# More buffers for the first pairs of attention, and a later start of a folded weight, in a fused retention and feed-forward kernel

## The reference

```python
scores = scale * np.matmul(q, k.transpose(0, 1, 3, 2))
Dmat = np.where(rel >= 0, gamma[:, None, None] ** rel[None, :, :], 0.0)
attn = np.matmul(scores * Dmat[None, :, :, :], v)
x = attn.transpose(0, 2, 1, 3).reshape(4608, 512)
h = np.maximum(np.maximum(x @ w1, x @ w2), x @ w3) @ w_out      # 512 -> 768 -> 512
return (((h @ u1) * (h @ u2)) @ u3) @ u_out                     # 512 -> 1024 -> 1024 -> 512
```

## Time and profile before

| | |
|---|---|
| median of three runs | 1245.4 us (1242.52 to 1248.57) |
| profiled execution | 1245.86 us, span 1244.1 us |
| PE busy | 1221.9 us, 98% of the span |
| DVE, ACT, POOL busy | 62%, 39%, 35% |
| attention (to the end of PE's values at 178.9 us) | 14% of the span |
| mean granted TensorE clock | 0.998 |

### The profile page before, as it was taken

The page is one execution under the profiler, slowest core; times in us unless marked ns, Lnnn a source line. Parts: engine busy times, 40 slices in busy tenths (PEclk is TensorE's granted clock), DMA queues, the critical chain, the costliest instruction groups (busy, mean ns, idle before and its releaser), DMA issues.

```text
span 1244.1 us, 21154 instructions
## 1 busy us (share of the span) xinstructions
PE 1221.9 (98%) x8288; PEld 1205.7 (97%) x8288; DVE 769.4 (62%) x1192; ACT 486.1 (39%) x779; POOL 435.3 (35%) x228
## 2 busy tenths in 40 slices
PE   7999999999999999999999999999999999999999
PEld 6999989999999999998999999999999999999998
DVE  6666857754546364657799668453545467875563
ACT  3433544423223232325555544242424243554441
POOL 2635529220100102051798562202020217265540
PEclk9999999999999999999999999999999999999999
DMA  9999954020302112052555541312131343444441
GB/s 341 331 328 333 309 166 159 33 96 27 102 27 82 46 56 72 27 171 80 198 202 190 171 155 55 109 52 102 51 109 57 109 153 125 153 152 160 152 159 65
DMA packets 88084, 169.96 MB, mean 137 GB/s; under 512 B 9904, under 2 KB 59184, under 8 KB 87984
## 3 DMA queue, kind: packets, MB, share of 16 engines
q1 hardware_dynamic: 87984, 168.60, 38.8%
HBM read 106.70 MB, written 61.87 MB: 135 GB/s over the span
## 4 chain that ended last, share of the span: by engine, by line
PE 85%; DVE 6%; DMA 3%; POOL 2%; issue 2%; SPq 1%; ACT 1%; DVEq 0%; ACTq 0%; POOLq 0%
PE ps L1075 25%; PE ps L1076 25%; PE ps L1077 25%; DVE wlo L807 2%; PE ps L975 2%; DVE clo L807 2%; PE ps L1023 2%; PE ps L1012 2%; POOL wraw L565 1%; DMA hd<-h 1%; PE ps L1038 1%; DMA xd<-xst 1%; PE ps L996 1%; PE ps L1042 1%; PE ps L1040 1%
## 5 line engine op out<-in xcount | busy, mean ns | idle before, releaser
L1075 PE MATMUL ps<-chi,whi 128*128 128x384 f32 x2016 | 675.4, 335 | 9.0 <-DVE h L897 6.4
L1077 PE MATMUL ps<-chi,wlo 128*128 128x384 f32 x2016 | 674.1, 334 | 0.0
L1076 PE MATMUL ps<-clo,whi 128*128 128x384 f32 x2016 | 674.0, 334 | 0.0
L565 POOL TENSOR_TENSOR raw<-raw,raw 128x768 f32<-128x768 f32 (+2 forms) x96 | 267.4, 2804 | 591.9 <-DMA raw<-xd 221.5
L1075 PEld LDWEIGHTS ps<-chi,whi 128*128 128x128 f32 x2016 | 378.9, 188 | 12.5 <-DVE h L897 8.3
L1076 PEld LDWEIGHTS ps<-clo,whi 128*128 128x128 f32 x2016 | 379.0, 188 | 0.0
L1077 PEld LDWEIGHTS ps<-chi,wlo 128*128 128x128 f32 x2016 | 378.8, 188 | 0.0
L807 DVE TENSOR_TENSOR clo<-raw,chi 128x768 fp32r<-128x768 f32 (+2 forms) x168 | 247.5, 1501 | 22.8 <-ACT chi L723 22.8
L723 ACT CAST chi<-raw 128x768 fp32r<-128x768 f32 (+2 forms) x168 | 180.5, 1081 | 85.1 <-PE ps L1077 61.7
L797 ACT COPY w<-ps 128x384 f32<-128x384 f32 x126 | 60.5, 480 | 249.8 <-PE ps L1077 248.3
L779 ACT COPY u<-ps 128x384 f32<-128x384 f32 x126 | 60.7, 482 | 159.2 <-PE ps L1077 155.8
(11 more groups left out here) (43 smaller groups left out, 838.5 us busy)
## 6 DMA issues: line engine op xcount, KB each, us to landing
qks<-qk SPq DMA_DIRECT2D x32, 576.0 KB, 6.5
gd<-h SPq DMA_DIRECT2D x96, 192.0 KB, 1.9
raw<-gd SPq DMA_DIRECT2D x24, 768.0 KB, 6.1
hd<-h SPq DMA_DIRECT2D x72, 192.0 KB, 1.9
raw<-hd SPq DMA_DIRECT2D x24, 576.0 KB, 5.7
x2d<-h SPq DMA_DIRECT2D x48, 192.0 KB, 2.4
raw<-x2d SPq DMA_DIRECT2D x24, 384.0 KB, 4.8
outT<-h SPq DMA_DIRECT2D x48, 192.0 KB, 1.9
```

Of the source, the lines that this page charges most:

```text
L565: return nc.gpsimd.tensor_tensor(out_, a, b, op)
L1075: nc.tensor.matmul(to, w1, x1, start=(start and k == 0), stop=False, skip_group_check=True)
L1076: nc.tensor.matmul(to, w1, x2, start=False, stop=False, skip_group_check=True)
L1077: last = nc.tensor.matmul(to, w2, x1, start=False, stop=(k == KH[st] - 1), skip_group_check=True)
```

## The change

Pairs 0 to 3 get buffers of their own for keys and state, and pairs 0 to 5 for queries and keys of the scores, in space that the second stage's weights use only later. More of the early loads therefore wait for nothing. In step 1 PE sums the state of each pair right after its scores (pair 3 in the PSUM bank of the folded weight), and DVE makes the state of pair 2 between the decays of pairs 2 and 3; in step 2 the state sums stand ahead of the queries. The folded weight begins in step 4: two quarters in steps 4 to 13, four in 14 to 16, and its loads, splits and reads move with it, some into places behind other loads of the same step. From pair 4 on the values of two pairs come in one load, and the tails of the values are loads of their own, two pairs each, for which PE waits before `values`. DVE clears four state buffers in place of two.

The diff, cut where it only puts `qk_buf(n)`, `k_buf(n)`, `v_buf(n)` or `state_buf(n)` in the place of a remainder, makes the buffers, or gives their semaphore counts:

```diff
-WC_FROM = 3
-QUARTERS = 4 * FT2
+QUARTERS = [0] * 4 + [2] * 10 + [4] * 3
...
+def qk_buf(n):
+    return n if n < 6 else n % 4
...
+def k_buf(n):
+    return n if n < 4 else n % 2
...
+def v_sem(n):
+    return n if n < 4 else (n - n % 2) % 6
...
+def state_buf(n):
+    return n if n < 4 else n % 2
...
-U3_LOAD = {min(2 * kb + WC_FROM - 2, STEPS - 3): kb for kb in range(FT2)}
-U3_SPLIT = {min(2 * kb + WC_FROM - 1, STEPS - 2): kb for kb in range(FT2)}
-UO_LOAD = {1: (0, 1), 2: (2, 3)}
-UO_SPLIT = {2: (0, 1), 3: (2, 3)}
-WC_READ = {min(2 * kb + WC_FROM + 1, STEPS - FT2 + kb): kb for kb in range(FT2)}
+U3_LOAD = {1: 0, 4: 1, 6: 2, 8: 3, 10: 4, 12: 5, 14: 6, 15: 7}
+U3_SPLIT = {3: 0, 5: 1, 7: 2, 9: 3, 11: 4, 13: 5, 14: 6, 15: 7}
+UO_LOAD = {2: (0, 1), 3: (2, 3)}
+UO_SPLIT = {3: (0, 1), 4: (2, 3)}
+WC_READ = {5: 0, 7: 1, 9: 2, 11: 3, 13: 4, 14: 5, 15: 6, 16: 7}
...
             def load_qk(n):
-                if n >= 4:
+                if n >= 6:
                     sp.wait_ge(scored, n - 3)
                     sp.wait_ge(q_decayed, n - 3)
...
+            def load_two_v(m):
+                n = 2 * m
                 if n >= 6:
-                    sp.wait_ge(valued, n - 5)
...
+                    sp.wait_ge(valued, n - 4)
+                sp.dma_start(vs[:, v_buf(n):v_buf(n) + 2, 0:NC * CH], vv[n:n + 2, :, :].rearrange("n p c -> p n c")
+                             ).then_inc(v_loaded[v_sem(n)], 16)
+
+            def load_tails(m):
+                n = 2 * m
+                sp.dma_start(vs[TAIL:P, v_buf(n):v_buf(n) + 2, NC * CH:], vt[n:n + 2, :, :].rearrange("n p c -> p n c")
+                             ).then_inc(vt_loaded[m % 3], 16)
...
             def load_k(n):
-                if n >= 2:
+                if n >= 4:
                     sp.wait_ge(state_summed, n - 1)
...
             load_v(1)
             load_k(1)
+            sp.dma_start(qtab[:, :, :], qdecay).then_inc(qtab_loaded, 16)
             load_qk(2)
-            sp.dma_start(qtab[:, :, :], qdecay).then_inc(qtab_loaded, 16)
+            load_decay(2, slice(4, HEADS))
+            load_k(2)
+            load_v(2)
             load_qk(3)
-            load_decay(2, slice(4, HEADS))
-            load_v(2)
+            load_k(3)
             load_v(3)
+            load_tails(0)
+            load_qk(4)
+            load_qk(5)
+            load_tails(1)
             for m in range(STEPS):
...
+                if m >= 2:
+                    if m in U3_LOAD:
+                        load_u3(U3_LOAD[m])
+                    if m in P1_W_LOAD:
+                        load_weight(P1_W_LOAD[m])
+                if m:
+                    for n in made_in(m + 1):
+                        load_k(n)
+                    if m in UO_LOAD:
+                        load_uo(UO_LOAD[m][0])
+                    for n in made_in(m + 2):
+                        load_qk(n)
+                    if m in UO_LOAD:
+                        load_uo(UO_LOAD[m][1])
+                    elif m == 1:
+                        load_u3(U3_LOAD[m])
+                if 2 * m + 4 < NP:
+                    load_two_v(m + 2)
+                    load_tails(m + 2)
+                for n in (2 * m - 2, 2 * m - 1):
+                    if n >= PAIRS:
+                        store_x(n)
...
             def make_state(n):
                 p = n % PAIRS
-                bank = S_WC if n == 1 else S_STATE
-                dve.wait_ge(state_summed, n + 2 - n % 2 if n >= 2 else n + 1)
+                bank = S_WC if n in (1, 3) else S_STATE
+                dve.wait_ge(state_summed, n + 2 - n % 2 if n >= 4 else n + 1)
...
             for m in range(STEPS):
                 for n in made_in(m):
                     decay_scores(n)
-                    if n == 0:
+                    if n in (0, 2):
                         make_state(n)
...
             def values(n):
                 pe.wait_ge(decayed, 3 * (n - n % 2 + 2))
+                pe.wait_ge(vt_loaded[n // 2 % 3], 16 * (n // 6 + 1))
...
             for m in range(STEPS):
                 for n in made_in(m):
                     scores(n)
-                    if m == 0:
+                    if m < 2:
                         sum_state(n)
                 for i in quarters(m):
                     wc_quarter(i)
+                for n in made_in(m) if m == 2 else ():
+                    sum_state(n)
                 for n in read_in(m):
                     query_state(n)
-                for n in made_in(m) if m else ():
+                for n in made_in(m) if m > 2 else ():
                     sum_state(n)
```

More of the change, by code:

```diff
@@ L177, in quarters, with qk_count, k_count, v_buf @@
 def quarters(m):
-    if m >= STEPS - 2:
-        return range(QUARTERS - 4 * (STEPS - m), QUARTERS - 4 * (STEPS - m) + 4)
-    return range(2 * (m - WC_FROM), 2 * (m - WC_FROM) + 2) if m >= WC_FROM else ()
-U3_LOAD = {min(2 * kb + WC_FROM - 2, STEPS - 3): kb for kb in range(FT2)}
-U3_SPLIT = {min(2 * kb + WC_FROM - 1, STEPS - 2): kb for kb in range(FT2)}
-UO_LOAD = {1: (0, 1), 2: (2, 3)}
-UO_SPLIT = {2: (0, 1), 3: (2, 3)}
-WC_READ = {min(2 * kb + WC_FROM + 1, STEPS - FT2 + kb): kb for kb in range(FT2)}
+    return range(sum(QUARTERS[:m]), sum(QUARTERS[:m + 1]))
+assert len(QUARTERS) == STEPS and sum(QUARTERS) == 4 * FT2
+def qk_buf(n):
+    return n if n < 6 else n % 4
+def qk_count(n):
+    return 16 if n < 6 else 16 * (n // 4 + (n % 4 > 1))
+def k_buf(n):
+    return n if n < 4 else n % 2
+def k_count(n):
+    return 16 if n < 4 else 16 * (n // 2)
+def v_buf(n):
+    return n % 6
+def v_sem(n):
+    return n if n < 4 else (n - n % 2) % 6
+def v_count(n):
+    return 16 if n < 4 else 16 * (n // 6 + 1)
+def state_buf(n):
[5 more added lines that the diff above has]
+WC_READ = {5: 0, 7: 1, 9: 2, 11: 3, 13: 4, 14: 5, 15: 6, 16: 7}
 P1_W_LOAD = {8: 0, 9: 1}
@@ L293, in build @@
         o += 2 * NC * CH * 4
-        state = [at(f"state{i}", [P, NC, P], f32, o + i * NC * P * 4) for i in range(2)]
+        state = [at(f"state{i}", [P, NC, P], f32, o + i * NC * P * 4 if i < 2 else first_at + (i - 2) * NC * P * 4)
+                 for i in range(4)]
+        first_at += 2 * NC * P * 4
+        assert first_at <= w_base[2]
         o += 2 * NC * P * 4
@@ L838, in make_state @@
                         if c == 0:
-                            nc.vector.tensor_copy(state[n % 2][own, c, own], new).then_inc(state_made, 1)
+                            nc.vector.tensor_copy(state[state_buf(n)][own, c, own], new).then_inc(state_made, 1)
                         else:
@@ L842, in make_state @@
                             nc.vector.scalar_tensor_tensor(
-                                state[n % 2][own, c, own], state[n % 2][own, c - 1, own], CHUNK_DECAY[2 * p + h], new,
-                                ALU.mult, ALU.add).then_inc(state_made, 1)
+                                state[state_buf(n)][own, c, own], state[state_buf(n)][own, c - 1, own],
+                                CHUNK_DECAY[2 * p + h], new, ALU.mult, ALU.add).then_inc(state_made, 1)
             def split_weight(wi, part):
@@ L974, in scores @@
                         keys = SEQ + c * CH
-                        nc.tensor.matmul(ps[:, 2 * (n % 2) + h, c * CH:(c + 1) * CH], qks[n % 4][own, keys:keys + CH],
-                                         qks[n % 4][own, c * CH:(c + 1) * CH],
+                        nc.tensor.matmul(ps[:, 2 * (n % 2) + h, c * CH:(c + 1) * CH], qks[qk_buf(n)][own, keys:keys + CH],
+                                         qks[qk_buf(n)][own, c * CH:(c + 1) * CH],
                                          start=(c == 0), stop=(c == NC - 1), skip_group_check=True)
@@ L1011, in query_state @@
                     bank, cols = x_cols(n, c)
-                    last = nc.tensor.matmul(ps[:, bank, cols], state[n % 2][:, c - 1, :],
+                    last = nc.tensor.matmul(ps[:, bank, cols], state[state_buf(n)][:, c - 1, :],
                                             qdec[n % 2][:, c - 1, 0:min(CH, SEQ - c * CH)],
@@ L1022, in values @@
                         own = slice(h * DH, h * DH + DH)
-                        last = nc.tensor.matmul(ps[own, bank, cols], vs[n % 6][:, c * P + h * DH:c * P + h * DH + DH],
+                        last = nc.tensor.matmul(ps[own, bank, cols], vs[:, v_buf(n), c * P + h * DH:c * P + h * DH + DH],
                                                 probs[n % 4][:, h, c * CH:min(SEQ, (c + 1) * CH)],
```

68 lines of the change are left out of this document (29 added, 39 removed).

## The result

The changed kernel takes 1260.8 us (median of five runs, 1257.7 to 1262.1) against 1245.4: 1.0117 of the time before, with a 95% interval of 1.0102 to 1.0132. It is some 15 us slower, where I forecast 1 us and allowed 5. The profiled execution took 1262.07 us for a span of 1260.3.

What follows compares the result with a forecast made beforehand. TensorE, busy 98% of the span, was taken to bound the kernel. The terms summed to +1.2 us on the profiled 1245.9, so 1247.1, or 1246.6 against the median 1245.4; range 1241 to 1251.

Steps and rivals of the forecast that it cites:

- Queue of loads, steps 0 to 2: First steps of attention: loads land at 382, then 366 kB per us; step 0 0 us, step 1 +0.5, step 2 -1.6.
- Step 3, +0.5: Step 3 without its two quarters: PE's two queries wait 0.5 us in all for DVE; bounds 0 and 1.3.
- Start of step 4, +1.5: Before scores 8: PE waits 1.5 us for ACT, held by a later `uo` load; bounds 0 and 2.6.
- Start of step 5, +1.1, at most 2.2: `load_uo(3)` behind q/k 11 and POOL's work: ACT ends at 52.2, PE ready at 51.1; bounds 0 and 2.2 us.
- Start of step 15, +1.0, at most 1.9: `u3` block 6 loaded and split in step 14: PE waits 1.0 us for `x_out` 27, between 0 and 1.9.
- rival in step 1: The pause in step 1 keeps PE at 1.2 GHz until step 2 begins; 1253.2 us, chance 0.05.
- Steps 5 to 12, 0: Middle of attention: no change, as PE has no idle there and work and order are unchanged.
- Steps 13 to 15, -1.8: End of attention: idle of 0.59, 0.80 and about 0.4 us goes; bounds 0 and -1.8.
- Every upper bound: The sum +1.2 us with the upper bounds added, given as +5.6 us or 1251, the top of the range.

Runs made afterwards that it cites:

- e8: Changed kernel with ACT splitting the second piece of `uo` behind the reads of the values, in steps 3 and 4; 1264.1 us.
- e12: Changed kernel with POOL decaying queries ahead of the `uolo` pieces in steps 3 and 4; 1253.0 us, 1.0059 of the kernel before.
- e10: Changed kernel unedited, run again for a second profile; 1260.5 us.
- e15: Changed kernel with the folded weight's whole old schedule, single value loads and step 2's state sums behind the queries, run again for another profile; 1247.7 us.
- e4: Kernel before with the first piece of `uo` loaded behind k and the second behind q/k; 1253.5 us, 1.0052 of the kernel before.
- e1: Changed kernel with both pieces of `uo` at the head of SP's list in steps 2 and 3; 1253.2 us, 1.0055 of the kernel before.
- e5: Changed kernel with the folded weight's whole schedule as in the kernel before; 1250.9 us, 1.0056 of the kernel before.
- e2: Changed kernel with `u3` blocks 6 and 7 loaded one step earlier; 1256.1 us, 1.0071 of the kernel before.
- e3: Changed kernel with `uo` at the head of SP's list and `u3` blocks 6 and 7 loaded one step earlier; 1250.1 us, 1.0032 of the kernel before.
- e13: Changed kernel with POOL's queries ahead of `uolo` in steps 3 and 4 and `u3` blocks 6 and 7 loaded one step earlier; 1248.2 us, 1.0018.

## Why the prediction was wrong

- **Queue of loads, steps 0 to 2**: right. Step 2 took 7.51 us (7.3 forecast), step 1 10.21 (10.6), and step 3 began at 30.95 (31.7). The cover of the two new memsets was just used up: PE's first wait is now ended by DVE, at 4.47.
- **Step 3, +0.5**: 0.9 (8.15 - 7.27), of which the queries' wait is 0.37.
- **Start of step 4, +1.5**: right in kind and size in the first profile: the second piece of `uo` reached ACT at 38.6 (39.0), PE waited 1.29. In the second profile it was 3.3, over my bound of 2.6.
- **Start of step 5, +1.1, at most 2.2**: the step that failed. The chain was the right one, and the issue time too (45.02, forecast 45.8), but I let 1.7 MB land by 50.4, 4.6 us at the 366 kB per us of the earlier trace rows. After SP's wait the queue moved 226 to 249 GB/s, the piece came at 53.4, and PE waited 4.4. The rate isn't all: from 44 to 53.4 the core moved about 2.4 MB (my estimate from the windows above), more than the 1.7 MB up to the piece, so transfers that stood behind it moved before it was complete. I had measured the queue only up to 37 us, while it was full. e8 adds that the stores of x were as late. e12 shows the chain: with POOL's order alone edited this pause is gone and 7.8 us come back.
- **Start of step 15, +1.0, at most 1.9**: failed in size. The issue was 8.9 us into the step, just as in the kernel before; I had taken 6.6, for a relief of POOL that didn't bring SP's list forward. The block was there 6.2 us later (6.0 forecast), ACT's read of the values followed, and PE waited 4.3.
- **The low clock behind a pause** had no term. I weighed it only as a rival in step 1, where it didn't occur. Behind the two long pauses it cost 1.5 us in step 5 (11.62 us busy for 10.1) and 1.75 in step 15 (14.92, where the kernel before is busy 13.17). The Trainium skill, TensorE: Matmul & The Clock Gate, "HAM oscillation — how this bites in real kernels", says that a long enough wait for DMA puts PE back to the low clock; the rows at 55.17 and 166.08, behind waits of 4.4 and 4.3 us, agree. The sum should have had a term for it behind each long wait.
- **Steps 5 to 12, 0**: 0.67 us in step 6, where ACT waited for a store, else right. **Steps 13 to 15, -1.8**: right in the first profile: but for the new pause PE has no idle in these steps (10.28, 12.92 and 14.92 us busy). It is small beside what came.
- **The range**: its upper end was added up wrongly. "Every upper bound" left out those of step 2 (+1.6), step 3 (+0.8) and steps 13 to 15 (+1.8); with them it is +9.8, or 1255, still under what was measured. The only rival that looked so far, a low clock in step 1, had another cause.

Together, by stretches against those of before with the quarters moved along: -1.8 up to step 3, then +0.9, +1.6, +5.8 and +0.9 in steps 3 to 6, 0 in steps 7 to 12, and +4.4 in steps 13 to 16 (4.3 of pause and 1.75 of slow clock, less the old idle). That is the 11.8 us by which attention is longer in the first profile; another 4.4 us lie behind attention, in the longer second wait and the low clock behind it; e10, the same kernel, has neither. In the second profile attention is 15.9 longer; the medians differ by 15.4.

## What to carry to other kernels

A load moved behind another in one in-order list inherits every wait of that list, and passes it on through each engine that waits in order: trace it through all of them (here POOL's query decay, SP, `uo`, ACT's reads, PE), and let the work that releases the list go first on its engine. Take a landing time from the stretch in question, not from the rate of a full queue elsewhere (8.4 us here where the full rate gave 4.6). Charge each new TensorE pause of a few us with the slow work that may follow it, 1.5 to 1.75 us here.

## What the runs showed of the hardware

- In attention, pauses of 1.5 to 2.5 us were followed by a granted clock of 0.50 in some places (1.51 us in e12, 1.80 in e15, 1.91 in e4, 2.15 in e1, 2.47 in e5) and not in others (1.85 in e2, 1.94 in e15, 2.05 in e3, 2.51 in e13). The pauses of 2.8 us and more (2.82 in e1 to 5.84 in e8) behind that for the first load all had it.
- The first matmuls behind a pause can still be fast, and the clock falls a little later. In e10 the first group behind pauses of 3.82 and 3.51 us took 1.16 us, not 2.08, but from 60 to 62 and from 172 to 175 the granted clock was about half. Timeline and windows of e10:

```profile
42.86 2.08 PE L1040 MATMUL ps<-qks 64*128 64x128 f32 x16 [3.33 <-ACT xst L746]
58.33 1.16 PE L1040 MATMUL ps<-qks 64*128 64x128 f32 x16 [3.82 <-ACT xst L746]
...
60.00:62.00 2.00, 2.00 (x19) 1.88 (x18) 1.16 (x3) 1.47 (x3) 2.00 (x3) 0.50 0.08 31
172.00:175.00 3.00, 3.00 (x26) 2.79 (x24) 2.08 (x4) 1.54 (x4) 2.56 (x3) 0.53 0.79 245
```

- The granted clock reads 1.00 in the first 18 us though the matmuls take twice their time until then. So it takes both signs: the length of equal matmuls at the start, the granted clock in windows of one or two us behind a pause.
- The same part of the program, 1065 us of it, varied by 7 us between executions (1062 to 1070), with two waits of PE and the low clock behind them. A profile of one execution says little on a difference of that size outside the part that was changed.
